# One-core attention and two gated layers: the first batch fed by head groups, the first tile's preparation spread over eleven steps, and another order of splits and loads in the layers

## The reference

```python
# q, k, v: (4 batches, 8 heads, 576 tokens, 64)
kv  = einsum('bhsd,bhse->bhde', k, v)
out = einsum('bhsd,bhde->bhse', q, kv)
x   = out / sqrt(mean(out*out, axis=-1) + 1e-6) * g_norm     # then 2304 tokens x 512
x   = ((x @ w_a) * (x @ w_b)) @ w_out                        # 512 -> 1536 -> 512
x   = (sigmoid(x @ w_gate) * (x @ w_val)) @ w_out2           # 512 -> 1536 -> 512
```

## Time and profile before

| | |
|---|---|
| time, median of 3 runs | 966.55 us (964.67 to 966.75) |
| the profiled execution's own time | 964.69 us |
| its span, first to last instruction | 962.9 us |
| PE busy (matmul) | 923.1 us, 96% of the span |
| DVE, ACT busy | 547.0 us (57%), 455.6 us (47%) |
| mean granted TensorE clock | 0.983 of full speed |

### The profile page before, as it was taken

One profiled execution on the slowest core, in us unless ns is written; L12 is line 12 of the kernel. 1 busy time (PEld: TensorE's weight loads), 2 busy tenths in 40 slices (PEclk: granted clock), 3 DMA queues, 4 the chain that ended last, 5 costly groups with the idle time before them and its releaser, 6 DMA issues.

```text
span 962.9 us, 14815 instructions
## 1 busy us (share of the span) xinstructions
PE 923.1 (96%) x5313; PEld 878.2 (91%) x5313; DVE 547.0 (57%) x1024; ACT 455.6 (47%) x931; POOL 16.8 (2%) x81
## 2 busy tenths in 40 slices
PE   7988889999999999999999999999999999999997
PEld 7878889998999999999999999987999988999986
DVE  1676867765455555455564777765455654545541
ACT  2555644545354534444444645454545454554531
POOL 1210100000000000000000000000000000000000
PEclk9978989999999999999999999999999999999999
DMA  9972065668354538445346456579535358554436
GB/s 232 250 184 79 23 224 170 217 207 314 136 197 142 187 134 282 139 167 189 140 156 205 134 173 197 186 251 346 181 144 195 131 205 273 179 183 145 154 109 197
DMA packets 85544, 177.13 MB, mean 184 GB/s; under 512 B 6368, under 2 KB 52448, under 8 KB 85472
## 3 DMA queue, kind: packets, MB, share of 16 engines
q1 hardware_dynamic: 85472, 176.19, 56.0%
HBM read 146.28 MB, written 29.88 MB: 183 GB/s over the span
## 4 chain that ended last, share of the span: by engine, by line
PE 80%; DVE 9%; DMA 4%; issue 3%; ACT 3%; SPq 1%; DVEq 0%; ACTq 0%
PE bank L566 47%; PE bank L602 14%; PE bank L600 13%; PE bank L499 2%; DVE w_lo L931 2%; PE bank L485 2%; DMA wo<-wo_dram 2%; DMA g_col<-in_g_norm_dram 1%; DVE c_b L1042 1%; DVE h_lo L951 1%; DVE c_b L1055 1%; DVE wo L945 1%; PE bank L511 1%; DMA w_raw<-in_moe_w_a_dram 1%; DVE h L1013 1%
## 5 line engine op out<-in xcount | busy, mean ns | idle before, releaser
L566 PE MATMUL bank<-x_hi,w_hi 128*128 128x384 f32 x1008 | 345.6, 343 | 12.8 <-ACT bank L797 5.4
L566 PE MATMUL bank<-x_hi,w_lo 128*128 128x384 f32 x1008 | 342.9, 340 | 0.0
L566 PE MATMUL bank<-x_lo,w_hi 128*128 128x384 f32 x1008 | 341.9, 339 | 0.0
L566 PEld LDWEIGHTS bank<-x_hi,w_hi 128*128 128x128 f32 x1008 | 190.5, 189 | 25.9 <-ACT bank L797 13.3
L566 PEld LDWEIGHTS bank<-x_lo,w_hi 128*128 128x128 f32 x1008 | 190.5, 189 | 6.1
L566 PEld LDWEIGHTS bank<-x_hi,w_lo 128*128 128x128 f32 x1008 | 190.5, 189 | 0.0
L741 ACT ACTIVATE h_hi<-h 128x384 fp32r<-128x384 f32 x144 | 74.6, 522 | 221.7 <-DVE h L1013 156.6
L600 PE MATMUL bank<-h_hi,wo 128*128 128x384 f32 x576 | 156.8, 336 | 3.3 <-DVE h_lo L951 1.5
L602 PE MATMUL bank<-wo,h_hi 128*128 128x512 f32 x432 | 139.6, 393 | 4.4 <-DVE h_lo L951 3.5
L931 DVE TENSOR_TENSOR w_lo<-w_raw,w_hi 128x512 fp32r<-128x512 f32 (+1 forms) x144 | 79.9, 555 | 106.4 <-ACT w_hi L707 105.8
L931 DVE TENSOR_TENSOR w_lo<-s_raw,w_hi 128x512 fp32r<-128x512 f32 x144 | 99.0, 688 | 71.6 <-ACT w_hi L707 71.5
(11 more groups left out here) (64 smaller groups left out, 739.4 us busy)
## 6 DMA issues: line engine op xcount, KB each, us to landing
wo<-wo_dram SPq DMA_DIRECT2D x120, 512.0 KB, 5.3
s_raw<-s_dram SPq DMA_DIRECT2D x48, 512.0 KB, 4.6
s_dram<-s_raw SPq DMA_DIRECT2D x24, 512.0 KB, 6.0
wo_dram<-wo SPq DMA_DIRECT2D x24, 512.0 KB, 3.9
w_raw<-in_moe_w_a_dram SPq DMA_DIRECT2D x18, 512.0 KB, 4.1
w_raw<-in_moe_w_b_dram SPq DMA_DIRECT2D x18, 512.0 KB, 3.6
w_raw<-in_moe_w_gate_dram SPq DMA_DIRECT2D x18, 512.0 KB, 3.8
w_raw<-in_moe_w_val_dram SPq DMA_DIRECT2D x18, 512.0 KB, 3.6
```

Of the source, the lines that this page charges most:

```text
L566: last = pe.matmul(to[:, 0:HT], w[:, u % 2, at, c, :], xx[:, i, c, :], start=(OPENS[i] and c == 0 and n_pass == 0), stop=(c == 1 and n_pas ...
```

## The change

Eight edits. (1) For batch 0 the head group is the outer index of the steps (`place_of`), each group's kv has its own bank (0 and 1) and is copied when its two pairs are done, both halves by ACT (`copy_kv`); SP loads two pairs' keys, then that group's queries. Pieces (0,2), (0,3) move behind `attend(0)` and `attend(1)`; the wait for g_norm stands behind `copy_q(1)`. (2) In batches 1 and 2 the pieces stand one step earlier, the kv copies one by one at steps 4 and 5, and the next batch's transposes around `transpose_x`. (3) Unit 0's weights are loaded ahead of batch 2's third pair. (4) The preparation of the first tile moves from steps 12 to 17 to steps 7 to 17, its last split into unit 0. (5) The late steps use three banks for `attend` in place of two, x's transposes bank 7 (4 for two of them). (6) In even units ACT's `split_h` goes behind the seed and one weight split. (7) In unit 11 `split_wo(10)`, `split_h(10)` and `last_h1` go earlier, two DVE weight splits behind `split_h(11)`; x's splits of the next tile start one step later. (8) SP: `load_unit` ahead of the raw out-weights, and unit 11's at projection step 21.

```diff
-    W_SUMS_AT, W_PREP_AT = 14, {15: (0, 1), 16: (2, 3)}
-    X_PREP_AT = {12: (0, 1), 13: (2,), 14: (3,), 15: (4,), 16: (5,), 17: (6,)}
-    KV_PIECE_AT = (None, None, 0, 1, 2, 3)
+    KV_PIECE_AT = [{0: (0, 2), 1: (0, 3), 2: (1, 0), 3: (1, 1), 4: (1, 2), 5: (1, 3)}] + [
+        {i + 1: (b + 1, i) for i in range(HEAD_PAIRS)} for b in range(1, BATCHES - 1)]
+    W_SUMS_AT = {7: (0, 1), 8: (2, 3)}
+    W_HI_AT, W_LO_AT = {7: (0,), 8: (1,), 9: (2,), 10: (3,)}, {7: (0,), 9: (1,), 10: (2,), 11: (3,)}
+    T_SUMS_AT = {11: (0,), 12: (1,), 14: (2,), 17: (3,)}
+    X_HI_AT = {8: (0,), 11: (1,), 12: (2,), 13: (3,), 14: (4,), 16: (5,)}
+    X_LO_AT = {9: (0,), 12: (1,), 13: (2,), 15: (3,), 16: (4,), 17: (5,)}
...
         def att_place(s):
-            return (2, 5, 6)[s % 3] if s < LATE else (5, 6)[s % 2]
+            return (2, 5, 6)[s % 3]
         def xT_place(s):
-            return 7 if s % 2 == 0 or s >= LATE - LAG else 1
+            return 4 if s in (ALL_STEPS - 3, ALL_STEPS - 1) else 7
...
+        def place_of(s):
+            b, i = divmod(s, STEPS)
+            if b == 0:
+                return b, i % (STEPS // HEAD_GROUPS) * 2, i // (STEPS // HEAD_GROUPS)
+            return b, i // HEAD_GROUPS * 2, i % HEAD_GROUPS
...
                     load_keys(b, pair_)
+                    if b == 2 and pair_ == 1:
+                        load_unit(0)
+                    if b == 0 and pair_ % 2:
+                        load_queries(0, pair_ // 2)
...
                     load_wo(n0 + v + 2)
+                    if v < UNITS - 1:
+                        load_unit(u + 3)
                     load_wo_raw(n0 + v + 1)
                     spill_wo(n0 + v - 1)
-                    load_unit(u + 3)
                 for i in range(12, STEPS_OF_TILE):
                     spill_wo(n0 + i - 1)
                     load_wo(n0 + i + 2)
+                    if i == 21:
+                        load_unit(unit(tau, UNITS) + 2)
...
                 if i == 0:
                     pe.wait_ge(w_lo_ready, 4 * u + 1)
                     if u == 0:
-                        pe.wait_ge(kv_upper_ready, BATCHES)
-                        pe.wait_ge(kv_lower_ready, BATCHES)
+                        pe.wait_ge(kv_lower_ready, HEAD_GROUPS * (BATCHES - 1) + 1)
...
-            for pair_ in range(HEAD_PAIRS):
-                keys_times_values(0, pair_)
             pe.wait_ge(identity_done, 1)
+            keys_times_values(0, 0)
+            keys_times_values(0, 1)
...
-            def copy_kv_upper(b):
-                act.wait_ge(kv_done, HEAD_PAIRS * (b + 1))
-                act.activation(kv[0:DH, b % 2, :, 0:DH],
-                               kv_bank[0:DH, :].rearrange("p (h e) -> p h e", e=DH),
+            def copy_kv(b, group):
+                heads = slice(group * GROUP, (group + 1) * GROUP)
+                act.wait_ge(kv_done, HEAD_PAIRS * b + 2 * (group + 1))
+                act.activation(kv[0:DH, b % 2, heads, 0:DH],
+                               kv_bank(group)[0:DH, heads_of(group)].rearrange("p (h e) -> p h e", e=DH),
                                ACT.Copy).then_inc(kv_upper_ready, 1)
+                act.activation(kv[DH:P, b % 2, heads, DH:P],
+                               kv_bank(group)[0:DH, heads_of(group)].rearrange("p (h e) -> p h e", e=DH),
+                               ACT.Copy).then_inc(kv_lower_ready, 1)
...
-            copy_kv_upper(0)
-            act.wait_ge(g_loaded, 32)
+            copy_kv(0, 0)
             copy_q(0)
             copy_q(1)
+            act.wait_ge(g_loaded, 32)
...
                 root(s)
+                if s == 1:
+                    copy_kv(0, 1)
+                if i == STEPS - 2:
+                    copy_kv(b + 1, 0)
+                if i == STEPS - 1:
+                    copy_kv(b + 1, 1)
...
                         act.activation(c_a[:, 1, :], product_bank(u - 1, BANK_B)[:, 0:HT], gate).then_inc(c21_a_ready, 1)
-                    elif v and (tau or v > 2):
-                        split_h(tau, v - 1)
...
                     split_w(u + 1, 0)
+                    if not b_unit and v and (tau or v > 2):
+                        split_h(tau, v - 1)
...
+                    if v == UNITS - 1:
+                        split_wo(tau, v - 1)
+                        split_h(tau, v - 1)
                     behind(v, 3)
...
                     behind(v, 4)
-                    split_w(u + 1, 2)
+                    if v == UNITS - 1:
+                        split_wo(tau, v - 1)
+                        split_h(tau, v - 1)
+                    else:
+                        split_w(u + 1, 2)
...
+                    if v == UNITS - 1:
+                        last_h1(PAIRS - 1)
...
-                    split_w(u + 1, 3)
+                    if v < UNITS - 1:
+                        split_w(u + 1, 3)
...
-                last_h1(PAIRS - 1)
...
                 split_wo(tau, CHUNKS - 1)
+                split_w(unit(tau, UNITS), 2)
+                split_w(unit(tau, UNITS), 3)
                 for q in range(CHUNKS, STEPS_OF_TILE):
                     split_h(tau, q)
                     if q == CHUNKS + 1:
                         drain(tau, 0)
-                    if tau + 1 < ALL_TILES and q - CHUNKS < 7:
-                        split_x(tau + 1, q - CHUNKS)
+                    if tau + 1 < ALL_TILES and 0 < q - CHUNKS <= 7:
+                        split_x(tau + 1, q - CHUNKS - 1)
```

More of the change, by code:

```diff
@@ L123, in attention_and_two_layers, with kv_bank, heads_of @@
         bank = [ctx.enter_context(nc.psum_tensor(f"bank{i}", [P, 512], F32)) for i in range(8)]
-        kv_bank = bank[0]
+        def kv_bank(group):
+            return bank[group]
+        def heads_of(group):
+            return slice(0, GROUP * DH)
         def qT_place(s):
@@ L396, in _ @@
                     load_keys(b, pair_)
+                    if b == 2 and pair_ == 1:
+                        load_unit(0)
+                    if b == 0 and pair_ % 2:
+                        load_queries(0, pair_ // 2)
                 if b == BATCHES - 1:
                     load_unit(1)
-                for group in range(HEAD_GROUPS):
-                    load_queries(b, group)
+                if b:
+                    for group in range(HEAD_GROUPS):
+                        load_queries(b, group)
                 if b == 0:
@@ L491, in attend @@
                 pe.wait_ge(qT_ready, s + 1)
[L492 to L494 removed]
+                pe.wait_ge(kv_lower_ready, HEAD_GROUPS * b + group + 1)
                 before = before_in_bank(att_place, s)
@@ L619, in _ @@
                 attend(s)
-                if KV_PIECE_AT[i] is not None:
-                    keys_times_values(b + 1, KV_PIECE_AT[i])
+                if i in KV_PIECE_AT[b]:
+                    keys_times_values(*KV_PIECE_AT[b][i])
                 if i + 2 < STEPS:
                     transpose_q(s + 2)
+                if i == STEPS - 1 and s + 1 < LATE:
+                    transpose_q(s + 1)
                 if s >= LAG:
@@ L679, in late @@
             def late(v, i):
+                if v == 0 and i == 0:
+                    split_x(0, 6)
                 if v == 0 and i in (1, 3, 5):
@@ L712, in split_x @@
                 elif tau == 0:
-                    act.wait_ge(x_ready, FIRST_TILE_STEPS)
+                    act.wait_ge(x_ready, STEPS if i in (0, 3) else FIRST_TILE_STEPS)
                 elif tau < TILES:
@@ L757, in _ @@
             act.activation(root_out[:, :], eps[:, :], ACT.Sqrt)
-            copy_kv_upper(0)
-            act.wait_ge(g_loaded, 32)
+            copy_kv(0, 0)
             copy_q(0)
             copy_q(1)
+            act.wait_ge(g_loaded, 32)
             for s in range(LATE):
                 b, i = divmod(s, STEPS)
-                for n in X_PREP_AT.get(s, ()):
-                    split_x(0, n)
                 square(s)
-                if i == STEPS - 1:
-                    copy_kv_upper(b + 1)
                 if i + 2 < STEPS:
                     copy_q(s + 2)
+                if i == STEPS - 1 and s + 1 < LATE:
+                    copy_q(s + 1)
                 if s >= LAG:
@@ L773, in _ @@
                 root(s)
-                for g in W_PREP_AT.get(s, ()):
+                if s == 1:
[4 more added lines that the diff above has]
+                    copy_kv(b + 1, 1)
+                if i == STEPS - 1 and s + 1 < LATE:
+                    copy_q(s + 2)
+                for g in W_HI_AT.get(s, ()):
                     split_w(0, g)
-                if i == STEPS - 1 and s + 1 < LATE:
-                    copy_q(s + 1)
-                    copy_q(s + 2)
+                for n in X_HI_AT.get(s, ()):
+                    split_x(0, n)
             for tau in range(ALL_TILES):
@@ L827, in _ @@
                             split_h(tau, q)
-                    elif v >= 2 or tau and v:
+                    elif v < UNITS - 1 and (v >= 2 or tau and v):
                         split_wo(tau, v - 1)
@@ L993, in _ @@
```

(22 more changed lines are left out.)

61 lines of the change are left out of this document (27 added, 34 removed).

## The result

The changed kernel takes 923.5 us (median of 4 runs, 923.11 to 924.99) against 966.65 before on the same occasions: ratio 0.956, 95% interval 0.9543 to 0.9577. The forecast was 928, a ratio of 0.960, with a range of 919 to 942. The profiled execution's span is 923.2, 39.7 under that of before; the sum of my terms was 38.2.

The account below looks back on a forecast made before the run. PE, busy for 96% of the span, was taken as the bound, so only its waits and low-clock stretches could be won. The terms summed to 38.2 us: 964.7 became 926.5, or 928 in the median's terms, range 919 to 942.

Parts of the forecast that it names:

- Start: Start of attention: third attend at 19.0 instead of 22.73, held by ACT's wait for g_col; 3.7 us gained.
- Between the batches: At both batch boundaries: PE's waits of 1.11 us each for both kv halves vanish; 2.2 us gained.
- both go: Two batch boundaries: with kv halves copied by group, the first a step earlier, both 1.11 us waits vanish.
- The transfers don't bound it, by some 3 us: Attention's loads: queue done at 58 us, PE needs the last piece at about 61.
- Preparation and gap: Steps 12 to 17 gain 5.5 us by spreading the first tile's preparation; the gap before unit 0 gains 3.0.
- Unit 0: Unit 0: its low-clock loss goes with PE busy up to the first product; 2.0 us gained, bounds 0 and 2.8.
- Late banks: Unit 1: with three banks attend waits for normalise of three steps before, not two; 2.8 us, bounds 1 and 4.
- Unit 4's weights: Unit 4's load, issued earlier, ends PE's 4.2 us stop and the low clock after; 6.2 us, bounds 4.2 and 6.5.
- Seeds: Unit pairs inside the tiles: split_h behind the seed removes PE's waits on it; 7.5 us, bounds 4 and 8.5.
- Unit 11: Six ends of unit 11: earlier splits remove waits on h_lo and loaded wo; 6.2 us, bounds 4 and 6.9.
- attention as long as it was fed: Rival, chance 0.22: DVE or the weights' load holds up steps 7 to 17, the 7.0 us return; 935.
- The low clock at the start: Rival without its own chance: PE works in bursts between landings at first, six slow operations; 931.

Follow-up runs that it names:

- x5_late: Changed kernel with ACT's split of x's sixth block at step 17, behind the last kv copy, instead of step 16; 923.87 us, ratio 0.9556.
- two_banks: Changed kernel with two banks for the late attends, as before the change, instead of three; 925.98 us, ratio 0.9587.
- prep_lump: Changed kernel with the first tile's preparation back in the old lumps at steps 12 to 16, only its last split in unit 0; 931.77 us, ratio 0.9638.
- g_first: Changed kernel with the two loads of g_col issued ahead of all others instead of behind batch 0; 926.93 us, ratio 0.959.
- start_old: Changed kernel with batch 0's old loads (all keys and values, then queries), pieces ahead of the transposes and joint kv copies, step order kept; 922.84 us, ratio 0.9551.
- w0_early: Changed kernel with unit 0's weights issued one key/value pair earlier, behind pair 0 of batch 2; 923.96 us, ratio 0.9564.
- seed_order_only: Kernel before with only ACT's split_h moved behind the seed and one weight split in even units; 954.65 us, ratio 0.9905.
- x5_and_transposes: Changed kernel with x's sixth split at step 17 and unit 2's last two transposes of x one product later; 922.21 us, ratio 0.9551.

## Why the prediction was right, point by point

**Start, 3.7 forecast, 3.4 seen: the number fits, the reason only in part.** The first attend came at 12.12 (12.4 estimated), ACT was let go at 18.02 and had copied the next q at 19.00, and the third attend came at 19.31.

```profile
12.12 2.02 PE L520 MATMUL bank<-kv,qT 128*96 128x128 f32 x8
...
18.02 0.59 ACT L692 ACTIVATE squares<-bank 96x512 f32<-96x512 f32 x1 [5.32 <-DMA g_col<-in_g_norm_dram]
18.52 0.48 ACT L678 ACTIVATE qT<-bank 128x384 f32<-128x384 f32 x1
...
19.31 1.04 PE L520 MATMUL bank<-kv,qT 128*96 128x128 f32 x8
```

But PE has no wait between 12.12 and 19.31, and the chain that ended last, which before went through g_col, now goes through PE's own work:

```profile
7.88 2.82 PE bank L504 x24
10.71 1.47 PE bank L491 x8
12.18 1.96 PE bank L520 x8
14.14 1.95 PE bank L504 x24
...
17.45 1.54 PE bank L504 x24
```

The first attend and the first piece took 2.02 us each here, where others take 1.04 and 1.61. Without that ACT would have been last, as it is elsewhere: in x5_late, two_banks and prep_lump PE waits 0.2, 0.6 and 1.0 us for the copied q, and the third attend is at 19.23, 18.65 and 18.81. So the 19.0 of the sum was right for ACT, and that PE's own work ends at the same time is luck. It goes with this that in g_first, where nobody waits for g_col, PE's own work alone took up to 19.09.

A part of the 3.4 is the clock, which the term didn't name. Before, PE had little to do from 14.4 to 18.6 and then ran at 0.59 up to the third attend; the changed kernel keeps 1.00 (a window of before, then one of the changed kernel, columns as in the earlier trace rows):

```profile
18.60:22.73 4.13, 4.13 (x25) 4.13 (x26) 0.88 (x2) 2.08 (x5) 0.59 (x3) 0.59 1.10 256
5.00:20.00 15.00, 14.91 (x135) 13.84 (x136) 0.88 (x2) 3.26 (x8) 0.19 (x1) 1.00 1.10 248
```

4.13 us at 0.59 are about 1.7 us lost, by my estimate.

The prediction took edit 1 as one, with the feed by head groups as its main part. The run start_old undid that feed, kept the gain at the third attend and had the same time. What it left in place is the wait for g_norm behind the two `copy_q` instead of ahead of them, the steps' order by head group, and the kv copies by ACT alone in two banks. Its rows show the first at work: both q are copied from 14.72 on, ahead of g_col's 16.89, where before they were copied at 18.04, behind it. The order by head group has a part too, since the second step no longer needs the second load of q, for which PE waited 1.6 us before, up to 17.54. By elimination the gain is of what is left; the wait's move alone was not run, so the shares stay argued.

**Between the batches, 2.2 forecast, 0.2 seen.** The failed step is "both go". The row that it rested on the earlier trace rows names ACT's copied q as what ended the wait, not a kv copy. The kv copies were indeed early, but the first boundary then waited for batch 1's queries (0.7), the second for ACT (0.9), which was behind with the preparation:

```profile
32.47 0.55 PE L491 MATMUL bank<-identity,q_in 96*128 96x96 f32 x4 [0.75 <-DMA q_in<-in_q_dram]
50.28 1.11 PE L520 MATMUL bank<-kv,qT 128*96 128x128 f32 x8 [0.90 <-ACT qT L678]
```

"The transfers don't bound it, by some 3 us" was wrong too: I compared the last piece's landing with PE's end, not each landing with its step. In g_first the stream was issued 1.3 us later and the time rose by more; in w0_early a later pair of batch 2 cost nothing that can be told. The price of a copied part was near enough: 0.36 and 0.38 us each, against the 0.40 of the nearest row.

**Preparation and gap, 5.5 + 3.0 forecast, and 0.9 taken off at the boundary.** Batch 2 and the gap gained 10.7, and with the 0.2 of the boundary it is 10.9 where these terms and the boundary gave 9.8. prep_lump shows what the spreading itself is worth: 4.5 us at the first product, 5.7 at unit 1 and 7.5 to 8 in the time, since the lump also lengthens the wait in unit 0. The rest, the gap and the copies by group, was not run alone. The fear that DVE would be 95% busy didn't come true: over both batches it was busy for 12.4 + 14.6 = 27.0 of 34.6 us, 78%, and unit 0 had 10.2 us of its work instead of 5.5. Unit 0's weights landed at 25.68 + 13.43 = 39.11, as forecast (39), and step 7 waited 0.5 us. They stand on the chain that ended last; w0_early took that wait away and gained nothing, with the values next in line.

```profile
25.68 13.43 DMA w_raw<-in_moe_w_a_dram
```

**Unit 0, 2.0 gained forecast, 2.0 lost.** The failed step is "with PE busy up to the first product". PE started product 0 at 67.53, but product 1 waited 1.67 for the second group's kv copy, and the clock went to 0.50 for the six us behind it (70.4 to 76.4). In this kernel's lines:

```profile
67.23 0.85 ACT L752 ACTIVATE x_hi<-x 128x768 fp32r<-128x768 f32 x1
67.98 0.57 ACT L692 ACTIVATE squares<-bank 96x512 f32<-96x512 f32 x1
...
69.90 0.38 ACT L686 ACTIVATE kv<-bank 64x256 f32<-64x256 f32 x1
70.42 0.66 PE L590 MATMUL bank<-x_hi,w_hi 128*128 128x384 f32 x1 [1.67 <-ACT kv L686]
```

attend(17) ended at 65.9, its square on ACT began at 67.98, and the copy is behind the root of that step. I had only asked for the first group's copy. The wait is the kernel's; the low clock is the single execution's: two_banks has the same wait of 1.7 and a clock of 1.00, unit 0 in 11.4 us. So without the low clock the term would have been 0, not -2.0: the higher clock takes PE's work from 11.4 us to 9.3, and PE's waits in the unit take it back.

**Late banks, 2.8 forecast, 2.3 seen, and 2.5 by two_banks.** Right, with a repayment that I hadn't named: unit 2's two transposes came before `normed` was ready (0.9).

**Unit 4's weights, 6.2 forecast, 6.5 seen**, 7.7 alone by the time, within its interval. Right.

**Seeds, 7.5 forecast, 10.5 seen, above my upper bound of 8.5.** The mechanism was right, as seed_order_only shows at every place; the size was off. One us of it is what I took off the 8.5 in case DVE was late, which it wasn't. The other 2: I used 19.07, layer 0's pair, as the floor for layer 1. The rows of the chain show the pairs of the changed kernel, tile 0, tile 3 (two pairs), tile 4:

```profile
135.17 2.12 PE bank L590 x12
154.24 2.12 PE bank L590 x12
...
546.15 3.12 PE bank L590 x18
564.98 3.12 PE bank L590 x18
...
675.19 3.12 PE bank L590 x18
694.03 3.12 PE bank L590 x18
```

Layer 0's pair is 19.07, layer 1's 18.83 or 18.84. So tile 3's pairs lost 0.86, not 0.63, and tiles 4 and 5 lost 0.2 a pair from unit 4 on, where I had counted none.

**Unit 11, 6.2 forecast, 8.0 seen, above the bound of 6.9.** I added up the waits listed, 6.9 us. One wait of 0.5 stays, for wo in a fresh tile, so 6.4 went, and the other 1.6 is some 0.27 an end: the size of the 0.25 of refill that I had counted for the seeds and forgotten here. That it is refill is argued, not shown.

Together: start -0.3, boundary -1.1, preparation and gap +2.2, unit 0 -4.0, banks -0.5, unit 4 +0.3, seeds +3.0, unit 11 +1.8, that is +1.4, and 38.2 became 39.7. In times the gain is 966.65 - 923.5 = 43.2 us, 3.5 more than in the profiled executions: that of before was 2.0 under its median, which I had counted, and that of the changed kernel was the slowest of its four (924.99), 1.5 above its median, with the low clock in unit 0. So the forecast was right in its sum and in most of its mechanisms, and the sum owes something to luck: what came out 5.9 us under its terms and what came out 7.3 us over them cancelled.

Of the rivals, attention as long as it was fed didn't come (10.9 us were won there), the seed's wait didn't move, and the raw out-weights weren't late. The low clock at the start isn't in the granted clock (1.00 from 5 to 20 us), though the first attend and piece were as slow as it would have made them. Of the signs, pairs of 19.07 in all tiles was wrong for layer 1 (18.83).

## What to carry to other kernels

Look at the start of each unit in both traces and at where the lead grows: it sorts a change of many edits better than any sum of waits, and it finds a floor that isn't one. A copy that is split in two halves needs both its due times looked at: the second half's consumer was one product later, and its engine was behind. A wait for a tiny load that stands at the head of an engine's order may be worth more than a new order of the large loads around it; undo the parts one by one before naming the one that pays. And where a forecast time comes out to 0.3 us, look at the chain that ended last: it may go through another engine than the one in the sum.

## Unexpected of the hardware

A wait of 1.7 or 1.8 us of PE in unit 0 was followed by a low clock in some executions and not in others. Over unit 0 the clock was 0.75 and 0.86 in the two profiled executions of the changed kernel, 0.74 in w0_early and 0.86 in g_first, but 1.00 in two_banks and start_old. After the shorter wait of 1.1 us, in x5_late and x5_and_transposes, it was 1.00 both times, and after the 3.9 us of prep_lump 0.77. The eight of these nine other than prep_lump show unit 0 between 11.1 and 13.4 us. The four runs of the changed kernel itself had a mean clock of 0.996, 1.000, 0.999 and 1.000 over the span, and the first was the slowest by 1.4 us. So up to 2 us of a time belong to the execution.

And at 12.12 an attend took 2.02 us instead of 1.04 with a granted clock of 1.00 in the records of that stretch. The same is in five of the nine profiled executions with this attention (both of the changed kernel, w0_early, x5_late, x5_and_transposes). In the other four PE had paused for 0.25 to 0.57 us just before, and the first attend took 1.11. Its cause stays open.
